# An attention and mixture-of-experts kernel: the second expert's weights move behind the first gathers, and the first value means come from a matmul

## The chip, the cores and the metric

The kernel runs on one core of a Trainium2 chip. The metric is the device time of one execution in microseconds (us), lower is better. TensorE, the matrix engine (PE in the profile), VectorE (DVE), ScalarE (ACT), GpSimd (POOL) and SyncE (SP) run their own instruction streams and wait for each other on semaphores. SP and POOL issue nearly all DMAs: SP's go through queue q1, POOL's through queue q0.

## The reference, cut to what matters

```python
# attention: B, H, S, D = 2, 8, 768, 64; block, window = 32, 16
k_sum = k.reshape(B, H, nb, block, D).max(axis=3)       # nb = 24 blocks
v_sum = v.reshape(B, H, nb, block, D).mean(axis=3)
# each query sees the keys less than 16 away, and 24 block maxima
# (their scores plus log(32)); softmax over both; values: v and v_sum
x = attention output as (1536, 512)
# mixture of experts: 8 experts, each token goes to its best two
for e in range(8):
    h = np.maximum(x[mask] @ w1[e], 0.0)        # w1[e]: 512 x 1024
    out[mask] += top2_w * (h @ w2[e])           # w2[e]: 1024 x 512
# then a dense layer: g = leaky(x @ w_in), g @ w_out, hidden width 2048
```

The block means of the values (`v_sum`) are what the change computes in another way for the first two heads. The two matrices of expert 1 are what it loads at another time.

## The kernel before, in words

**Attention.** Two heads make a pair; there are eight pairs (n = 0 to 7), each in three groups of four units of 64 queries (c = 3n + g). For a pair, SP loads the queries (L281), the keys (L285), the value windows with their two halos (L293 to L295) and the block means of the values (L302). PE transposes queries and keys into one shared bank, `turned` (L1044, L1053), and ACT and DVE copy them out (L612, L791, L617). For each group PE forms scores (L1066), DVE adds masks and takes maxima, ACT takes exponentials, PE transposes the probabilities (L1075) and multiplies them with the value windows (`weigh`, L1090), whose last 24 rows are the block means. Results go to the memory tensor `x_tokens` (L318).

**Block means.** For all heads they come from three loads of 128 rows of 8 KB (`load_rows`, L306) into the staging buffer `stage`, from five halving adds on POOL each (`block_means`, L465, L467), and from a store to memory (`store_means`, L311). `load_means` (L302) reads them back, broadcast over the twelve units. So the first `weigh` waits for rows, adds, a store and a load.

**SP** works through one hand-written list. A wait in it holds back every DMA that is written behind it.

**POOL** has one list too: constants, three `block_means`, the weights of expert 0, then (after the fifth transposed key pair) the weights of expert 1, a few constants, and the wait for the routing (`token_of_done`). `load_weights` brings one expert's two matrices in eight pieces of 512 KB through four slots of `stage` and splits each into a high and a low half (L495 and L497), 4 pieces for w1 (then `w1_ready`, L500) and 4 for w2 (then `w2_ready`). Two buffers of split weights exist: even experts use buffer 0, odd ones buffer 1.

**Routing.** Between attention and the experts, a chain mostly on DVE finds for each slot of each tile of 128 its token (`token_of`).

**Experts.** POOL gathers the token rows of tiles 0 to 2 straight into `x_first` (L548) and those of the others through a ring of seven slots into a memory tensor sorted by tile (gather L538, store L529, the store four tiles behind its gather). It gathers tiles up to 23, loads expert 2, gathers two tiles, loads expert 3, gathers the last five, and loads the others in a loop. PE runs the tiles in order: transposes, the second product of tile t-2, and the first product of tile t, which waits for `w1_ready` of its expert (L1190 is the matmul line of both products). After the experts comes the dense layer (L1274 to L1291).

Of the kernel before, what the change touches and what calls it, by code (L numbers as in the profile page):

```python
# [25 lines left out]
P = 128  # L26
# [9 lines left out]
KC = WK + NB  # L36
VC = D + 1
AT = P
MASKED = -1e9
EPS = 1e-9  # L40

# [25 lines left out]
def build(nc, q, k, v, w_gate, w_noise, noise, w1, w2, w_in, w_out, out):  # L67
    ctx = ExitStack()
    with ctx:
        def sem(name):  # L70
            return ctx.enter_context(nc.semaphore(name))

        def sb(name, shape, dt=F32, where=ctx):
            return where.enter_context(nc.sbuf_tensor(name, shape, dt))
# [32 lines left out]
        with ExitStack() as room:  # L107
            qk_nat = sb("qk_nat", [P, 2, TPB, 2, D], where=room)
            q_diag = sb("q_diag", [P, 2, UNITS, 2 * QB], where=room)
            kT = sb("kT", [P, 2, UNITS, KC], where=room)  # L110
            k_max = sb("k_max", [P, NB], where=room)
            v_win = sb("v_win", [KC, 2, 2, UNITS, VC], where=room)
            masks = sb("masks", [P, GROUPS - 1 + GU, KC], where=room)
            scores = sb("scores", [P, 2, GU, KC], where=room)
            probs = scores
            xT_gate = sb("xT_gate", [P, S], where=room)
            v_mean = xT_gate[:, 0:3 * D].rearrange("p (i d) -> p i d", i=3)
            negmax = sb("negmax", [P, 2, GU], where=room)
# [62 lines left out]
        zeros_done = sem("zeros_done")  # L181
# [39 lines left out]
        o_bank = [p67[:, 512 * i:512 * i + GU * VC].rearrange("x (u c) -> x u c", u=GU) for i in range(2)]  # L221
        gate_bank = [p67[:, 512 * i + GU * VC:512 * i + GU * VC + GM] for i in range(2)]
        last_gate_bank = p23[:, 0:GM]
        rank_bank = p01[:, 0:NT * E]
        count_bank = p23[:, 0:E]
        token_bank = p23[:, 512:512 + TCOLS]
# [51 lines left out]
        def _(sp):  # L278
# [24 lines left out]

            def load_rows(i):

                sp.dma_start(stage[:, 2 * (i % 2):2 * (i % 2) + 2, :].rearrange("p a n -> p (a n)"),  # L306
                             v_rows[i * P:(i + 1) * P, :]).then_inc(v_nat_loaded[i], 16)

            def store_means(i):
                sp.wait_ge(v_mean_done, i + 1)  # L310
                sp.dma_start(vsum_dram[i * P:(i + 1) * P, :], v_mean[:, i, :]).then_inc(v_mean_stored[i], 16)  # L311

            def store_x(n, g):

# [5 lines left out]

            load_q(0)
            load_k(0)
            load_rows(0)
            sp.wait_ge(consts_done, 2)
            load_windows(0)
            sp.wait_ge(q_turned, 1)
            load_q(1)
            sp.wait_ge(k_turned, 1)
            load_k(1)
            load_rows(1)  # L330
            sp.wait_ge(q_turned, 2)
            load_q(2)
            load_windows(1)
            store_means(0)
            load_rows(2)
            sp.wait_ge(v_mean_stored[0], 16)
            load_means(0)
            load_means(1)
            for n in range(PAIRS):
                if n + 2 < PAIRS:  # L340
                    sp.wait_ge(k_turned, n + 2)
                    load_k(n + 2)
                if n >= 1:
                    store_x(n - 1, 0)
                    if n + 1 < PAIRS:
                        sp.wait_ge(weighed, GROUPS * n)
                        load_windows(n + 1)
                        load_means(n + 1)
                    store_x(n - 1, 1)
                    store_x(n - 1, 2)  # L350
                if n + 3 < PAIRS:
                    sp.wait_ge(q_turned, n + 3)
                    load_q(n + 3)
                if n == 0:
                    for i in (1, 2):
                        store_means(i)
                    for i in (1, 2):
                        sp.wait_ge(v_mean_stored[i], 16)
            sp.wait_ge(k_turned, PAIRS)
            sp.dma_start(noise_sb[:], noise.rearrange("(t p) e -> p t e", p=P)).then_inc(noise_loaded, 16)  # L360
            for g in range(GROUPS):
# [56 lines left out]
        def _(pool):  # L418
# [20 lines left out]
            link(pool.memset(v_win[0:WINDOW, :, 0, 0, 0:D], 0.0))  # L439
            signal(pool.memset(v_win[64:WK, :, 1, UNITS - 1, 0:D], 0.0))  # L440

            link(pool.memset(masks[:, :, WK:KC], math.log(BLOCK)))
            link(pool.memset(masks[:, :, 0:WK], 0.0))
            units = GROUPS - 1 + GU
# [13 lines left out]

            def block_means(i):

                rows = stage[:, 2 * (i % 2):2 * (i % 2) + 2, :].rearrange("p a n -> p (a n)")
# [5 lines left out]
                pool.tensor_scalar(v_mean[:, i, :], rows[:, 0:D], 1.0 / BLOCK, 1.0, ALU.mult, ALU.mult).then_inc(v_mean_done, 1)  # L467

            def settled():

# [33 lines left out]
            pool.wait_ge(v_mean_done, 3)  # L504
            settled()
            load_weights(lambda c: weight_piece(0, c), 0, 0, reused=False)
            pool.wait_ge(k_turned, 5)
            load_weights(lambda c: weight_piece(1, c), 1, 1, reused=False)


            pool.wait_ge(k_turned, PAIRS)
# [78 lines left out]
        def _(act):  # L590
# [41 lines left out]
            q_part(0)  # L632
            k_part(0)
            k_means(0)
            q_part(1)
            for n in range(PAIRS):
                c = GROUPS * n
                if c >= 1:
                    probs_out(c - 1)
                softmax_exp(c)  # L640
                if n + 1 < PAIRS:
                    k_part(n + 1)

                probs_out(c)
                softmax_exp(c + 1)
                if n >= 2:
                    if n == 2:
                        for i in range(3):
                            act.wait_ge(v_mean_stored[i], 16)
                    act.wait_ge(gate_turned, n - 1)  # L650
                    act.wait_ge(gate_multiplied, n - 2)
                    gate_xT(n - 2)

                probs_out(c + 1)
                if n + 1 < PAIRS:
                    k_means(n + 1)
                softmax_exp(c + 2)
                if n + 2 < PAIRS:
                    q_part(n + 2)
# [77 lines left out]
        def _(dve):  # L737
# [70 lines left out]
            q_part(1)  # L808
            dve.wait_ge(consts_done, 3)
            for n in range(PAIRS):  # L810
                for g in range(GROUPS):
                    c = GROUPS * n + g
                    if c >= 3:
                        normalise(c - 3)
                    softmax_max(c)
                    if g == 1 and n + 1 < PAIRS:
# [14 lines left out]
            dve.wait_ge(consts_done, 5)  # L831
# [203 lines left out]
        def _(pe):  # L1035
# [42 lines left out]
            def weigh(c):  # L1078

                b = c % 2  # L1080
                n, g = divmod(c, GROUPS)
                if g == 0:
                    pe.wait_ge(v_loaded[n % 2], 80 * (n // 2 + 1))
# [12 lines left out]
            def gate_turn(m, first=0, end=TPB):  # L1096

# [19 lines left out]
            pe.wait_ge(zeros_done, 1)  # L1117
            turn_q(0)
            turn_k(0)
            turn_q(1)  # L1120
            for n in range(PAIRS):
                c = GROUPS * n
                score(c)
                if c >= 1:
                    turn_probs(c - 1)
                if n + 1 < PAIRS:
# [5 lines left out]
                turn_probs(c)  # L1132
                if n >= 2:
                    gate_turn(n - 2)
                if c >= 1:
# [205 lines left out]
```

## Time and profile before

| | |
|---|---|
| median of 3 runs | 835.51 us (832.05 to 835.52) |
| profiled execution | 829.91 us, its span 828.3 us |
| attention, to the last logits | 0 to 130.2 us of the span |
| routing | 130.2 to 153.1 us |
| first matmul of an expert | 159.26 us |
| last split of expert 1 | ends at 115.1 us |
| weight load of expert 2 | begins at 208.34 us |
| dense layer begins | about 550 us |

The times of the rows are microseconds from the start of the span, in one profiled execution. PE busy is the matrix engine's own busy time, PEclk its granted clock (1.00 is 2.4 GHz, 0.50 is 1.2 GHz), and the DMA share is that of 16 DMA engines.

### The profile page before, as it was taken

To read this page: it belongs to the slowest core of one execution; us is meant where nothing else is said; L and a number is where in the kernel's file an instruction comes from. 1 tells how busy PE (TensorE), PEld (TensorE's weight loads), DVE (VectorE), ACT (ScalarE), POOL (GpSimd) and SP (SyncE) were. 2 spreads that over 40 slices of the span, in tenths; PEclk is the share of its full clock that TensorE was granted. 3 is DMA by queue.
4 is the path that set the end of the run, shared out by engine and by line. 5 is a ranking of instruction groups with operands and counts; after the bars stand their busy time and mean duration, and the time that the engine had idled before them with its cause. 6 is when DMAs were issued, how large, how long until landed. Compare 5 with 4: busy or idle time off the path is not lost.

```text
span 828.3 us, 12304 instructions
## 1 busy us (share of the span) xinstructions
PE 754.7 (91%) x4026; PEld 632.2 (76%) x4027; DVE 272.5 (33%) x521; ACT 224.1 (27%) x405; POOL 392.5 (47%) x350
## 2 busy tenths in 40 slices
PE   3569892699999999999999999979999999999997
PEld 3458782578878888888888888878788887888885
DVE  3456556321221221222222122136343324432223
ACT  2557562022112212112112121225222222222221
POOL 5687860465786967888788783610011001000000
PEclk9889895599999999999999999989999999999999
DMA  9799970389726364353444441334011101010001
GB/s 213 177 286 227 268 128 13 112 288 297 242 89 215 127 214 173 120 187 143 144 142 156 138 141 38 114 127 154 13 39 51 51 1 50 0 51 0 0 1 51
DMA packets 87422, 103.15 MB, mean 125 GB/s; under 512 B 55680, under 2 KB 61824, under 8 KB 86976
## 3 DMA queue, kind: packets, MB, share of 16 engines
q0 software_dynamic: 17008, 59.52, 22.0%
q1 hardware_dynamic: 69328, 43.22, 20.5%
q8 instruction: 17, 0.28, 0.2%
q10 hardware_dynamic: 1056, 0.03, 0.1%
q14 instruction: 13, 0.11, 0.0%
HBM read 80.89 MB, written 23.69 MB: 126 GB/s over the span
## 4 chain that ended last, share of the span: by engine, by line
PE 61%; POOL 13%; DMA 10%; SPq 7%; DVE 4%; issue 4%; ACT 1%; POOLq 0%; DVEq 0%
PE p L1190 23%; POOL w_lo L497 6%; PE p L1274 5%; PE p L1276 5%; PE p L1275 5%; PE p L1289 5%; PE p L1291 5%; PE p L1290 5%; DMA x_by_tile<-x_ring 3%; POOL w_hi L495 3%; SPq L294 2%; DMA x_ring<-x_tokens,token_of 2%; POOL x_ring L538 2%; PE p L1182 2%; DMA stage<-in_moe_w 2%
## 5 line engine op out<-in xcount | busy, mean ns | idle before, releaser
L497 POOL TENSOR_TENSOR w_lo<-stage,w_hi 128x1024 fp32r<-128x1024 f32 x72 | 171.8, 2386 | 6.0
L1190 PE MATMUL p<-w_hi,xT_hi 128*128 x248 | 100.1, 404 | 3.3 <-DVE xT_lo L929 1.6
L584 POOL DMA_INDIRECT y_pick<-y_by_tile,slots x20 | 19.1, 955 | 165.9 <-PE p L1261 150.2
L1190 PE MATMUL p<-w_lo,xT_hi 128*128 x248 | 97.2, 392 | 0.0
L1190 PE MATMUL p<-w_hi,xT_lo 128*128 x248 | 97.2, 392 | 0.0
L1190 PE MATMUL p<-w_hi,hT_hi 128*128 x240 | 96.5, 402 | 0.0
L1190 PE MATMUL p<-w_lo,hT_hi 128*128 x240 | 93.9, 391 | 0.0
L1190 PE MATMUL p<-w_hi,hT_lo 128*128 x240 | 93.5, 390 | 0.0
L495 POOL TENSOR_SCALAR w_hi<-stage 128x1024 fp32r<-128x1024 f32 x72 | 75.9, 1054 | 18.9 <-DMA stage<-in_moe_w 14.8
L1274 PE MATMUL p<-f_xT_hi,w_hi 128*128 (+2 forms) x200 | 78.3, 392 | 1.3 <-DVE f_xT_lo L978 1.3
L1275 PE MATMUL p<-f_xT_lo,w_hi 128*128 (+2 forms) x200 | 77.2, 386 | 0.0
L1276 PE MATMUL p<-f_xT_hi,w_lo 128*128 (+2 forms) x200 | 77.1, 386 | 0.0
L1289 PE MATMUL p<-w_hi,f_hT_hi 128*128 128x512 f32 x192 | 75.0, 390 | 1.4 <-DVE f_hT_lo L988 1.3
L1291 PE MATMUL p<-w_hi,f_hT_lo 128*128 128x512 f32 x192 | 74.7, 389 | 0.0
L1290 PE MATMUL p<-w_lo,f_hT_hi 128*128 128x512 f32 x192 | 74.7, 389 | 0.0
L686 ACT CAST hT_hi<-p 128x1024 fp32r<-128x1024 f32 x30 | 30.5, 1015 | 156.5 <-PE p L1182 143.3
L929 DVE TENSOR_TENSOR xT_lo<-p,xT_hi 128x512 fp32r<-128x512 f32 x31 | 21.4, 692 | 154.6 <-ACT xT_hi L683 149.9
L986 DVE SCALAR_TENSOR_TENSOR f_h<-p,f_h 128x512 f32<-128x512 f32 x48 | 33.2, 691 | 116.6 <-ACT f_h L708 116.6
L681 ACT ACTIVATE h_row<-p 128x1024 f32<-128x1024 f32 x30 | 30.8, 1027 | 139.7 <-PE p L1190 134.6
L708 ACT COPY f_h<-p 128x512 f32<-128x512 f32 x48 | 28.2, 588 | 142.2 <-PE p L1276 142.2
L935 DVE COPY y_row<-p 128x512 f32<-128x512 f32 x31 | 21.5, 693 | 115.6 <-PE p L1190 115.6
L476 POOL DMA_DIRECT2D stage<-in_moe_w x64 | 41.5, 650 | 33.0 <-POOL w_lo L497 22.5
(184 smaller groups left out, 1253.8 us busy)
## 6 DMA issues: line engine op xcount, KB each, us to landing
stage<-in_moe_w POOLq DMA_DIRECT2D x64, 512.0 KB, 4.9
y_by_tile<-y_row SPq DMA_DIRECT2D x31, 256.0 KB
x_by_tile<-x_ring POOLq DMA_DIRECT2D x28, 256.0 KB, 6.9
x_row<-x_by_tile SPq DMA_DIRECT2D x28, 256.0 KB
qk_nat<-in_q SPq DMA_DIRECT2D x16, 192.0 KB, 5.6
qk_nat<-in_k SPq DMA_DIRECT2D x16, 192.0 KB, 4.7
stage<-in_v SPq DMA_DIRECT2D x3, 1024.0 KB, 7.8
v_win<-in_v SPq DMA_DIRECT2D x8, 384.0 KB
```

The source lines that it names most:

```text
L476: pool.dma_start(stage_view(c % STAGES, c), source(c)).then_inc(staged[c % STAGES], 16)
L495: pool.tensor_scalar(w_hi[:, par, cols], stage[:, c % STAGES, :], 1.0, 1.0, ALU.mult, ALU.mult).then_inc(hi_split, 1)
L497: pool.tensor_tensor(w_lo[:, par, cols], stage[:, c % STAGES, :], w_hi[:, par, cols].bitcast(F32), ALU.subtract).then_inc(lo_split, 1)
L681: nc.scalar.activation(h_row[:], h_bank[:], ACT.Relu).then_inc(h_ready, 1)
L986: nc.vector.scalar_tensor_tensor(out=h, in0=f_h_bank[c % 2], scalar=0.01, in1=h, op0=ALU.mult, op1=ALU.max).then_inc(f_leaky_done, 1)
L1190: last = nc.tensor.matmul(bank, a, w, start=(c == 0 and i == 0), stop=(c == left_hi.shape[1] - 1 and i == 2))
L1274: nc.tensor.matmul(to, hi, f_xT_hi[:, cols], start=(k == 0), stop=False)
L1275: nc.tensor.matmul(to, hi, f_xT_lo[:, cols], start=False, stop=False)
L1276: last = nc.tensor.matmul(to, lo, f_xT_hi[:, cols], start=False, stop=(k == KD - 1))
L1289: nc.tensor.matmul(f_y_bank[m], f_hT_hi[:, c % 2, rows], hi, start=(c == 0), stop=False)
L1290: nc.tensor.matmul(f_y_bank[m], f_hT_hi[:, c % 2, rows], lo, start=False, stop=False)
L1291: last = nc.tensor.matmul(f_y_bank[m], f_hT_lo[:, c % 2, rows], hi, start=False, stop=(c == FC - 1))
```

## The change

1. The weights of expert 1 are loaded (and split) after the gathers of tiles 0 to 9, and no longer during attention. The gathers of tiles 10 to 23 and everything that POOL does after them come behind that load.
2. The block means of the first pair (`n = 0`) come from twelve accumulating matmuls of a 0-or-1/32 matrix (`in_block`) with the value windows, and one ScalarE copy that broadcasts them into the window tile. The first 48 rows of means are no longer summed on POOL, and `load_means(0)` is gone. The three row loads are now of 128, 128 and 80 rows (`MEAN_ROWS`).
3. The order of the first loads on SP and of the first turns on PE, ACT and DVE: the second pair's queries turn after the first scores, its keys after the first probabilities; row loads 1 and 2 come later, and the stores of means 1 and 2 (with SP's waits for them) move into the later rounds of the loop, ahead of `load_means(n + 1)`.

```diff
+MEAN_ROWS = [(2 * NB, 2 * NB + P), (2 * NB + P, 2 * NB + 2 * P), (2 * NB + 2 * P, B * H * NB)]
...
 (SyncE)
             load_q(0)
             load_k(0)
-            load_rows(0)
             sp.wait_ge(consts_done, 2)
             load_windows(0)
             sp.wait_ge(q_turned, 1)
             load_q(1)
+            load_rows(0)
             sp.wait_ge(k_turned, 1)
             load_k(1)
-            load_rows(1)
+            load_windows(1)
             sp.wait_ge(q_turned, 2)
             load_q(2)
-            load_windows(1)
             store_means(0)
-            load_rows(2)
+            load_rows(1)
             sp.wait_ge(v_mean_stored[0], 16)
-            load_means(0)
             load_means(1)
             for n in range(PAIRS):
...
+                if n == 0:
+                    load_rows(2)
...
                         load_windows(n + 1)
+                        if n < 3:
+                            store_means(n)
+                            sp.wait_ge(v_mean_stored[n], 16)
                         load_means(n + 1)
...
-                if n == 0:
-                    for i in (1, 2):
-                        store_means(i)
-                    for i in (1, 2):
-                        sp.wait_ge(v_mean_stored[i], 16)
...
 (GpSimd)
+            link(pool.memset(in_block[:], 0.0))
+            blocks = in_block[:, NB - 2:NB]
+            link(pool.memset(blocks, 1.0 / BLOCK))
+            link(pool.affine_select(out=blocks, ...))
+            signal(pool.affine_select(out=blocks, ...))
...
             load_weights(lambda c: weight_piece(0, c), 0, 0, reused=False)
-            pool.wait_ge(k_turned, 5)
-            load_weights(lambda c: weight_piece(1, c), 1, 1, reused=False)
...
-            gather_tiles(FIRST, 2 * NT)
+            gather_tiles(FIRST, FIRST + RING)
+            load_weights(lambda c: weight_piece(1, c), 1, 1, reused=False)
+            gather_tiles(FIRST + RING, 2 * NT)
             pool.wait_ge(table_done, 1)
             load_weights(lambda c: weight_piece(2, c), 2, 0)
...
 (ScalarE, after softmax_exp(0))
+                if n == 0:
+                    act.wait_ge(first_means_done, 1)
+                    nc.scalar.copy(v_win[WK:KC, 0, :, :, 0:D], first_mean_bank ... broadcast over UNITS).then_inc(first_means_ready, 1)
+                    q_part(1)
...
 (TensorE)
+            def first_means():
+
+                pe.wait_ge(v_loaded[0], 48)
+                pe.wait_ge(consts_done, 3)
+                for u in range(UNITS):
+                    last = nc.tensor.matmul(first_mean_bank, in_block[:, NB - 2 - 2 * u:2 * NB - 2 - 2 * u], v_win[0:WK, 0, :, u, 0:D],
+                                            start=(u == 0), stop=(u == UNITS - 1))
+                last.then_inc(first_means_done, 1)
...
             turn_q(0)
             turn_k(0)
-            turn_q(1)
             for n in range(PAIRS):
                 c = GROUPS * n
                 score(c)
...
-                if n + 1 < PAIRS:
+                if n == 0:
+                    first_means()
+                    turn_q(1)
+                elif n + 1 < PAIRS:
                     turn_k(n + 1)
...
                 score(c + 1)
                 turn_probs(c)
+                if n == 0:
+                    turn_k(1)
```

## Rows read from the trace of the kernel before

**Rows 1.** The page, busy time of the engines over the span.
```profile
PE 754.7 (91%) x4026; PEld 632.2 (76%) x4027; DVE 272.5 (33%) x521; ACT 224.1 (27%) x405; POOL 392.5 (47%) x350
```
**Rows 2.** Busy time by stretch: stretch, length, engines, then clock, DMA share, GB/s.
```profile
0.00:130.20 130.20, 92.68 (x912) 82.52 (x913) 66.78 (x148) 67.87 (x155) 88.07 (x93) 0.91 0.96 209
...
230.40:330.50 100.10, 98.75 (x484) 81.97 (x482) 21.16 (x25) 20.45 (x25) 77.19 (x63) 1.00 0.48 163
330.50:828.30 497.80, 485.16 (x2264) 402.55 (x2264) 151.00 (x236) 117.74 (x203) 174.68 (x135) 0.99 0.24 80
```
**Rows 3.** Timeline of PE, first products of tiles 0, 3, 6, 14; start, duration.
```profile
159.26 0.79 PE L1190 MATMUL p<-w_hi,xT_hi 128*128 x1 [1.60 <-DVE xT_lo L929]
...
162.69 0.40 PE L1190 MATMUL p<-w_lo,xT_hi 128*128 x1
...
193.58 0.48 PE L1190 MATMUL p<-w_hi,xT_hi 128*128 x1
...
231.74 0.49 PE L1190 MATMUL p<-w_hi,xT_hi 128*128 x1 [1.00 <-POOLq L500]
...
330.50 0.49 PE L1190 MATMUL p<-w_hi,xT_hi 128*128 x1 [0.35 <-POOLq L500]
```
**Rows 4.** Timeline of POOL, from the first gather to the load of expert 2.
```profile
153.09 1.06 POOL L548 DMA_INDIRECT x_first<-x_tokens,token_of  x1 [36.26 <-DVE token_of L925]
...
165.75 0.98 POOL L538 DMA_INDIRECT x_ring<-x_tokens,token_of  x1 [0.30 <-issue]
...
167.62 0.98 POOL L538 DMA_INDIRECT x_ring<-x_tokens,token_of  x1 [0.30 <-issue]
...
193.05 0.97 POOL L538 DMA_INDIRECT x_ring<-x_tokens,token_of  x1 [4.89 <-DMA x_by_tile<-x_ring]
...
200.77 0.97 POOL L538 DMA_INDIRECT x_ring<-x_tokens,token_of  x1 [0.30 <-DMA x_by_tile<-x_ring]
...
208.34 1.60 POOL L476 DMA_DIRECT2D stage<-in_moe_w  x3
```
**Rows 5.** Groups of POOL instructions, 150 to 210 us: count, busy, mean; idle before.
```profile
L538 POOL DMA_INDIRECT x_ring<-x_tokens,token_of x21 | 20.3, 967 | 15.4 <-DMA x_by_tile<-x_ring 10.8 <-issue 4.6
L529 POOL DMA_DIRECT2D x_by_tile<-x_ring x21 | 12.2, 580 | 3.8 <-DMA x_ring<-x_tokens,token_of 3.8
```
**Rows 6.** Timeline of POOL: ends of expert 1's load, and of expert 2's.
```profile
76.07 2.19 POOL L476 DMA_DIRECT2D stage<-in_moe_w  x4 [0.61 <-POOL w_lo L497]
...
112.77 2.36 POOL L497 TENSOR_TENSOR w_lo<-stage,w_hi 128x1024 fp32r<-128x1024 f32 x1
...
229.09 2.37 POOL L497 TENSOR_TENSOR w_lo<-stage,w_hi 128x1024 fp32r<-128x1024 f32 x1
...
247.90 1.06 POOL L538 DMA_INDIRECT x_ring<-x_tokens,token_of  x1 [0.83 <-POOL w_lo L497]
```
**Rows 7.** DMA queues in 0:102.5, then 76:102.5 (two rows), then 37:50: packets, MB, share.
```profile
q1 hardware_dynamic: 48427, 15.98, 80.1%
...
q1 hardware_dynamic: 12639, 3.54, 77.7%
q0 software_dynamic: 1016, 3.70, 40.7%
...
q1 hardware_dynamic: 3926, 1.05, 42.2%
```
**Rows 8.** The chain that ended last, in time: the last key load.
```profile
95.34 7.16 DMA qk_nat<-in_k
```
**Rows 9.** Timeline of PE in attention: turn, first product with values, scores.
```profile
16.25 1.54 PE L1044 MATMUL p<-ident,qk_nat 128*128 128x128 f32 x6 [7.23 <-DMA qk_nat<-in_q]
...
32.41 1.19 PE L1090 MATMUL p<-v_win,probsT 120*64 120x65 f32 x16 [6.30 <-DMA v_win<-v_means]
...
69.29 1.15 PE L1066 MATMUL p<-kT,q_diag 128*128 128x120 f32 x8
...
79.61 1.15 PE L1066 MATMUL p<-kT,q_diag 128*128 128x120 f32 x8
```

More of the change, by code:

```diff
@@ L117, in build @@
             v_mean = xT_gate[:, 0:3 * D].rearrange("p (i d) -> p i d", i=3)
+            in_block = xT_gate[0:WK, 3 * D:3 * D + 2 * NB - 2]
             negmax = sb("negmax", [P, 2, GU], where=room)
@@ L180, in build @@
         v_loaded = [sem(f"v_loaded{i}") for i in range(2)]
-        zeros_done = sem("zeros_done")
+        zeros_done = sem("zeros_done"); first_means_done = sem("first_means_done"); first_means_ready = sem("first_means_ready")
         q_turned = sem("q_turned"); k_turned = sem("k_turned")
@@ L223, in build @@
         last_gate_bank = p23[:, 0:GM]
+        first_mean_bank = p67[WK:KC, 512:512 + 2 * D]
         rank_bank = p01[:, 0:NT * E]
@@ L304, in load_rows @@
             def load_rows(i):
-                sp.dma_start(stage[:, 2 * (i % 2):2 * (i % 2) + 2, :].rearrange("p a n -> p (a n)"),
-                             v_rows[i * P:(i + 1) * P, :]).then_inc(v_nat_loaded[i], 16)
+                first, end = MEAN_ROWS[i]
+                sp.dma_start(stage[0:end - first, 2 * (i % 2):2 * (i % 2) + 2, :].rearrange("p a n -> p (a n)"),
+                             v_rows[first:end, :]).then_inc(v_nat_loaded[i], 16)
             def store_means(i):
+                first, end = MEAN_ROWS[i]
                 sp.wait_ge(v_mean_done, i + 1)
-                sp.dma_start(vsum_dram[i * P:(i + 1) * P, :], v_mean[:, i, :]).then_inc(v_mean_stored[i], 16)
+                sp.dma_start(vsum_dram[first:end, :], v_mean[0:end - first, i, :]).then_inc(v_mean_stored[i], 16)
             def store_x(n, g):
@@ L440, in _ @@
             signal(pool.memset(v_win[64:WK, :, 1, UNITS - 1, 0:D], 0.0))
+            link(pool.memset(in_block[:], 0.0))
+            blocks = in_block[:, NB - 2:NB]
+            link(pool.memset(blocks, 1.0 / BLOCK))
+            link(pool.affine_select(out=blocks, in_=blocks, compare_op=ALU.is_ge, fill=0.0, base=-WINDOW, pattern=[[-BLOCK, 2]], channel_multiplier=1))
+            signal(pool.affine_select(out=blocks, in_=blocks, compare_op=ALU.is_ge, fill=0.0, base=WINDOW + BLOCK - 1, pattern=[[BLOCK, 2]], channel_multiplier=-1))
             link(pool.memset(masks[:, :, WK:KC], math.log(BLOCK)))
@@ L459, in block_means @@
             def block_means(i):
-                rows = stage[:, 2 * (i % 2):2 * (i % 2) + 2, :].rearrange("p a n -> p (a n)")
+                first, end = MEAN_ROWS[i]
+                rows = stage[0:end - first, 2 * (i % 2):2 * (i % 2) + 2, :].rearrange("p a n -> p (a n)")
                 pool.wait_ge(v_nat_loaded[i], 16)
@@ L466, in block_means @@
                     half //= 2
-                pool.tensor_scalar(v_mean[:, i, :], rows[:, 0:D], 1.0 / BLOCK, 1.0, ALU.mult, ALU.mult).then_inc(v_mean_done, 1)
+                pool.tensor_scalar(v_mean[0:end - first, i, :], rows[:, 0:D], 1.0 / BLOCK, 1.0, ALU.mult, ALU.mult).then_inc(v_mean_done, 1)
             def settled():
@@ L634, in _ @@
             k_means(0)
-            q_part(1)
             for n in range(PAIRS):
@@ L640, in _ @@
                 softmax_exp(c)
-                if n + 1 < PAIRS:
+                if n == 0:
+                    act.wait_ge(first_means_done, 1)
+                    nc.scalar.copy(v_win[WK:KC, 0, :, :, 0:D], first_mean_bank.rearrange("x (h d) -> x h d", h=2).unsqueeze(2).to_broadcast([NB, 2, UNITS, D])).then_inc(first_means_ready, 1)
+                    q_part(1)
+                elif n + 1 < PAIRS:
                     k_part(n + 1)
@@ L645, in _ @@
                 softmax_exp(c + 1)
+                if n == 0:
+                    k_part(1)
                 if n >= 2:
@@ L807, in _ @@
             k_blocks(0)
-            q_part(1)
-            dve.wait_ge(consts_done, 3)
+            dve.wait_ge(consts_done, 4)
             for n in range(PAIRS):
@@ L815, in _ @@
                     softmax_max(c)
-                    if g == 1 and n + 1 < PAIRS:
+                    if c == 0:
+                        q_part(1)
+                    if c == 2:
+                        k_blocks(1)
+                    if g == 1 and 1 <= n < PAIRS - 1:
                         k_blocks(n + 1)
@@ L830, in _ @@
             dve.wait_ge(noise_loaded, 16)
-            dve.wait_ge(consts_done, 5)
+            dve.wait_ge(consts_done, 6)
             dve.wait_ge(logits_added, PAIRS + 1)
@@ L1081, in weigh @@
                 n, g = divmod(c, GROUPS)
-                if g == 0:
-                    pe.wait_ge(v_loaded[n % 2], 80 * (n // 2 + 1))
+                if c == 0:
+                    pe.wait_ge(first_means_ready, 1)
+                if g == 0 and n >= 1:
+                    pe.wait_ge(v_loaded[n % 2], (80 if n % 2 else 48) + 80 * (n // 2))
                 pe.wait_ge(probsT_ready, c + 1)
@@ L1125, in _ @@
                     turn_probs(c - 1)
-                if n + 1 < PAIRS:
+                if n == 0:
+                    first_means()
+                    turn_q(1)
+                elif n + 1 < PAIRS:
                     turn_k(n + 1)
@@ L1132, in _ @@
                 turn_probs(c)
+                if n == 0:
+                    turn_k(1)
                 if n >= 2:
```

## The prediction

> **What bounds the kernel now.** I read the page first: PE is busy 91% of the span, POOL 47% [rows 1]. That average hides three stages, so I went on to the busy time by stretch. In attention, the first 130.2 us, PE is busy 92.7 us; the DMA share is 0.96 [rows 2]. From 230.4 us on PE has almost no gap: 98.75 of 100.1 us, then 485.2 of 497.8 us, the gaps of the latter being in the dense layer [rows 2]. Whatever delays PE at about 230 us therefore delays the end by the same amount; nothing later takes it up.
>
> Next the timeline of PE at the start of each expert. The first product of tile 6 starts at 231.74 us, after 1.00 us of waiting for POOL's L500, the signal that an expert's w1 is split; tile 14 waits 0.35 us at 330.50 us for the same line [rows 3]. So tile 6 is the first of expert 2 (POOL's load that ends its fourth split at 229.09 + 2.37 = 231.5 us is the one begun at 208.34 us [rows 4, 6]). Experts 0 and 1 have six tiles, and POOL's chain (gathers, expert 2, expert 3, expert 4) is exactly as long as PE's, with no slack at all at two places. That is the fact on which the forecast rests: **work added to POOL between 153 and 208 us is work added to the end.**
>
> In attention the question is what ends the waits. The chain that ended last runs through SP's DMAs and their landings up to the last key load, 95.34 + 7.16 = 102.5 us [rows 8]; from there 27.7 us remain to 130.2. Up to 102.5 us q1 is busy 80.1%, 82.1 us [rows 7]: attention is paced mainly by SP's queue of small packets.
>
> **The load of expert 1 behind the gathers.** I follow POOL from its first gather, 153.09 us, in times of before.
>
> Block one, the gathers of tiles 0 to 9: the last starts at 165.75 us [rows 4], 12.7 us in. Then its remaining stores must wait for their gathers to land. The same tail before, from the last gather at 200.77 us to the load at 208.34, is 7.6 us [rows 4]. Sum 20.2 us.
>
> The load itself: from 208.34 to the next gather at 247.90 us, 39.6 us [rows 4, 6]; in attention expert 1 took 76.07 to 115.13, 39.1 us [rows 6]. POOL splits in order, so none of this lies beside other POOL work. I take 39.6, with up to 41.0 if DMA is crowded.
>
> Block two, the gathers of tiles 10 to 23: before, from 167.62 to 208.34, 40.7 us [rows 4]. Four of the stores in it (tiles 6 to 9, 0.58 us each [rows 5]) now belong to block one: 38.4. It held ring waits: 10.8 us in six, against 0.3 us that every gather has, 9.0 us too much; one was 4.89 us [rows 4, 5]. After the load the ring is empty, and a gather meets its slot's store three gathers after it was issued. I keep three waits of 1.2 us, 3.5 us: 32.9 us. Low: no ring waits; high: all of them, 38.4. The tail waits (3.8 us [rows 5]) may partly go in both blocks, 2.2 us each at the low end.
>
> Sum: 20.2 + 39.6 + 32.9 = 92.7 us, against 208.34 - 153.09 = 55.3 before. Expert 2's load starts **37.5 us later** against the end of routing; low 18.0 + 39.6 + 27.2 = 84.8 (+29.6), high 20.2 + 41.0 + 38.4 = 99.6 (+44.4).
>
> What is late next: the first product of tile 3, the first of expert 1, stands at 193.58 us [rows 3]; its w1 would be ready 23.2 us (208.34 to 231.5) after 173.3, at 196.5, so PE waits 3 us there. The wait at tile 6 swallows it: PE is ready at about 234 and starts at 269, some 35 us idle. From there POOL needs 122.2 us from expert 2's load to expert 4's w1, as before (208.34 to 330.5), and PE needs its eight tiles of 12.3 us [rows 3] too, so the delay neither grows nor shrinks. The clock adds a little: after the idle of routing the first eight matmuls took 159.26 to 162.69, 3.4 us, instead of the 1.8 that they take at the pace of a tile, 48 products and twelve short transposes in 12.3 us, some 0.23 us each [rows 3]. The idle at tile 6 should cost the same 1.6 us, less the 0.6 us by which tile 14 was late anyway: **+1.0 us**. Bounds 0 and 2.
>
> **What attention gives back.** In 76 to 102.5 us, with expert 1's weights beside it, q1 is busy 77.7%, idle 5.9 us [rows 7]. Without those weights I give that back in full: 5.9. The 576 packets of `load_means(0)` at 82.1 x 16 / 48427 = 27.1 ns are 1.0 us of the 16 engines; the 48 rows not loaded, 0.39 MB, are about 1.2 us at the rate of 0.96 DMA share [rows 2, 7]. Sum 2.2. The hole from 37 to 50 us, where q1 is busy only 42.2%, 7.5 us idle [rows 7], comes where SP stands at the stores of means 1 and 2 before it loads keys; these now come later, but SP now stands at `store_means(0)` for the same sums and meets the others in rounds 1 and 2, each ahead of `load_means` and of a whole round of loads. I count half, 3.8. Together **G = 12 us**.
>
> The early waits, 7.23 us for queries before the first scores and 6.30 us for `v_means` before the first `weigh` [rows 9], both go; but they are waits on the queue that paces the whole stage, and taking them away only lets PE reach the next load sooner. They are not added. The new matmuls cost under 1.2 us (16 of L1090 took 1.19 [rows 9]) and the copy little more, hidden by the loads of pair 1. The four small POOL constants are hidden by the wait for the first rows. PE now waits for windows 0 before it turns the second queries, and behind that stand the keys of pair 1; between 0 and 5 us if those windows are late.
>
> Bounds of G: at most q1 without gaps, 82.1 - 2.2 + 2.3 of start = 82.2 instead of 102.5: 20.3. At least 0.
>
> A rule speaks to the 5.9. The Trainium skill, DMA: Bandwidth & Descriptors, section Queues, rings and completion order, says that each DMA engine takes turns between the queue rows that have work, a packet at a time. Then each weight packet held q1 back by its own time, 40.7% of 26.5 us = 10.8 us [rows 7], where the idle share gives 5.9; by it G is 16.9 and the time 5 us less.
>
> **The sum.** 829.9 (the profiled execution; its span is 828.3) + 37.5 + 1.0 - 12 = 856.4. The median of the runs, 835.5, stands 5.6 above that execution; the middle of all four times is 832.7, and with +26.5 it gives **859 us**.
>
> **Rivals.**
> - **Attention gives more back**, G from 15 to 20: the turns between queues, or the hole goes fully. For it: the 10.8 us above. Against it: it needs an SP that stands nowhere, and each round has waits for `weighed` and `x_ready` in front of the next windows. Time with G = 17 to 20: 851 to 854. Chance 0.18.
> - **The change does not do what it says in attention**, G under 7: SP stands behind the sums of means, or behind the windows, and the freed DMA time is idle. For it: the hole at 37 to 50 us is of this kind and is only moved. Time with G = 2: 869. Chance 0.14.
> - **Not slower**, through one mechanism: q1's price per packet falls once the weights are gone. With q1 gapless (G = 20.3) a further 18 us are needed, 48427 packets falling from 27.1 to 21 ns. In 37 to 50 us they took 5.5 x 16 / 3926 = 22.4 ns [rows 7], but those were another mix. At 20 ns G is 42 and the time 829. Against it too: attention would have to end at about 92 us, with PE busy for 92.7 [rows 2], while an undisturbed pair takes 79.61 - 69.29 = 10.3 us [rows 9]. Faster 0.04, same 0.02.
>
> My forecast's own case (G 7 to 15) has 0.62. The range: with G = 20.3 and +29.6 it would be 843, with G = 5 and +44.4 it would be 873; both ends at once are unlikely, so 847 to 870. What this measurement can tell from no change is about 0.5%, 4 us. Slower: 0.94.
>
> **What would show it.** PE idle of 30 to 40 us before tile 6's first product, put down to L500, and PEclk at half there; POOL's eight splits of expert 1 between the gathers; the routing's end about 12 us earlier, near 141 us; q1 above 85% from 76 us on; the first scores at about 12 us. I would be wrong if PE's wait at tile 6 were under 25 us (block two much quicker), or if routing ended before 130 us.

## The result and the profile after

The changed kernel takes **867.3 us** (median of 4 runs, 863.5 to 869.0) against 835.5 (832.1 to 837.2): a ratio of 1.038, 95% interval 1.033 to 1.043. It is slower, by 31.8 us in the medians. The profiled execution took 863.45 us, its span 861.9, which is 33.6 more than the span before.

The page after, busy time and its 40 slices (21.5 us each), then the group that POOL holds up:

```profile
PE 758.8 (88%) x4050; PEld 634.3 (74%) x4051; DVE 272.7 (32%) x521; ACT 225.2 (26%) x406; POOL 393.8 (46%) x354
...
PE   5829973889707999999999999988999999999997
...
PEclk9869985899957999999999999998999999999999
...
L1223 PE MATMUL p<-w_hi,xT_hi 128*128 x248 | 101.6, 410 | 38.1 <-POOLq L510 36.1
```

PE has only 4.1 us more to do than in [rows 1], but its share falls from 91 to 88%. The twelfth slice (237 to 259 us), an idle PE at half its clock, is the one to explain: it lies just ahead of expert 2's tiles. The same by stage (columns as in [rows 2]):

```profile
0.00:125.50 125.50, 93.49 (x936) 82.15 (x937) 66.82 (x148) 69.02 (x156) 56.37 (x73) 0.90 0.91 179
125.50:148.40 22.90, 6.87 (x30) 6.55 (x30) 19.49 (x97) 3.35 (x5) 0.00 (x0) 0.50 0.00 1
148.40:264.30 115.90, 73.51 (x340) 60.01 (x340) 15.65 (x18) 15.68 (x19) 85.94 (x84) 0.81 0.64 211
264.30:365.00 100.70, 100.67 (x484) 83.81 (x485) 19.66 (x23) 19.73 (x24) 76.62 (x63) 0.98 0.49 159
365.00:861.90 496.90, 484.22 (x2262) 401.82 (x2260) 151.03 (x236) 117.47 (x203) 174.82 (x135) 0.99 0.24 80
```

The last two stretches stand for the last two of [rows 2] and are within 1 us of them. All of the loss is in the third: from the end of routing to tile 6 it was 231.74 - 153.09 = 78.65 us, and is 115.9 now. Attention gives 4.65 us back. PE's waits, summed, name the two places:

```profile
PE p L1223 <- POOLq L510: 36.1, 2, 32.8
PE p L1062 <- ACT xT_gate L637: 15.4, 1, 15.4
...
PE p L1062 <- DMA qk_nat<-in_q: 4.9, 1, 4.9
```

Columns: total, times, longest. The first row is the forecast wait (L510 is the old L500, L1223 the old L1190). The second was not forecast.

**POOL, where the forecast lay.** Its timeline, to be held against [rows 4] and [rows 6]:

```profile
148.44 1.06 POOL L556 DMA_INDIRECT x_first<-x_tokens,token_of  x1 [47.97 <-DVE token_of L943]
...
161.08 0.99 POOL L546 DMA_INDIRECT x_ring<-x_tokens,token_of  x1 [0.30 <-issue]
...
168.33 2.13 POOL L486 DMA_DIRECT2D stage<-in_moe_w  x4
...
208.97 1.07 POOL L546 DMA_INDIRECT x_ring<-x_tokens,token_of  x1 [0.79 <-POOL w_lo L507]
...
239.13 1.61 POOL L486 DMA_DIRECT2D stage<-in_moe_w  x3
...
261.71 2.34 POOL L507 TENSOR_TENSOR w_lo<-stage,w_hi 128x1024 fp32r<-128x1024 f32 x1
```

Block one is 148.44 to 168.33 = 19.9 us, the load 40.6, block two 30.2; together 90.7 against 55.25 before: +35.4. Expert 2's first weights then take 24.9 us to `w1_ready` (23.2 before). PE's timeline:

```profile
192.98 0.79 PE L1223 MATMUL p<-w_hi,xT_hi 128*128 x1 [3.35 <-POOLq L510]
...
264.33 0.79 PE L1223 MATMUL p<-w_hi,xT_hi 128*128 x1 [32.79 <-POOLq L510]
...
267.86 0.40 PE L1223 MATMUL p<-w_lo,xT_hi 128*128 x1
```

Tile 3 waits 3.35 us and tile 6 32.79 us; the next eight products take 3.5 us instead of 1.8, at a granted clock of 0.51, the lower of the two levels. That is [rows 3] moved by 37.2 us against the end of routing.

**Attention, where it did not lie.** SP and then ScalarE at the second wait:

```profile
53.91 0.47 SPq L298 DMA_DIRECT2D v_win<-in_v  x1
54.42 0.46 SPq L316 DMA_DIRECT2D v_means<-xT_gate  x1
61.43 0.76 SPq L305 DMA_DIRECT2D v_win<-v_means  x2
```

```profile
61.55 0.80 ACT L637 COPY xT_gate<-p 128x768 f32<-128x768 f32 x1 [15.78 <-issue]
```

The sums of means (`v_mean`) lie in the memory of `xT_gate`. So before ScalarE writes the first `xT_gate` it waits for all three stores of means. The third store stands in round 2 of SP's list now, behind the windows of the next pair and what those wait for; it is issued at 54.42, and SP's wait for its landing ends by 61.4. Until then ScalarE stands for 15.8 us and PE for 15.4. The idle is labelled "issue" on ScalarE: only the code and SP's timeline say what it was.

### The profile page after: what moved, and what is told of

Its sections match the earlier page's. It is cut to its first block, busy times and chain, and to the rows that moved or that the text cites. A ratio compares the mean times of both kernels' runs of the same rounds, so it can differ in the third digit from the quotient of the medians.

```text
span 861.9 us, 12355 instructions
## 1 busy us (share of the span) xinstructions
PE 758.8 (88%) x4050; PEld 634.3 (74%) x4051; DVE 272.7 (32%) x521; ACT 225.2 (26%) x406; POOL 393.8 (46%) x354
## 3 DMA queue, kind: packets, MB, share of 16 engines
q0 software_dynamic: 17008, 59.52, 21.5%
q1 hardware_dynamic: 68632, 42.66, 19.9%
## 4 chain that ended last, share of the span: by engine, by line
PE 74%; POOL 8%; DMA 7%; issue 4%; DVE 4%; ACT 1%; SPq 1%; DVEq 0%; POOLq 0%; ACTq 0%
PE p L1223 33%; PE p L1307 5%; PE p L1308 5%; PE p L1309 5%; PE p L1322 5%; PE p L1323 5%; PE p L1324 5%; POOL w_lo L507 3%; PE p L1215 3%; PE p L1084 2%; DMA x_by_tile<-x_ring 2%; PE p L1110 2%; POOL w_hi L505 1%; POOL x_ring L546 1%; DMA stage<-in_moe_w 1%
## 5 line engine op out<-in xcount | busy, mean ns | idle before, releaser
L1223 PE MATMUL p<-w_hi,xT_hi 128*128 x248 | 101.6, 410 | 38.1 <-POOLq L510 36.1
L1223 PE MATMUL p<-w_hi,xT_lo 128*128 x248 | 98.5, 397 | 0.0
L1223 PE MATMUL p<-w_lo,xT_hi 128*128 x248 | 98.3, 396 | 0.0
L1223 PE MATMUL p<-w_hi,hT_hi 128*128 x240 | 96.5, 402 | 0.0
L1223 PE MATMUL p<-w_lo,hT_hi 128*128 x240 | 93.9, 391 | 0.0
L1223 PE MATMUL p<-w_hi,hT_lo 128*128 x240 | 93.5, 390 | 0.0
L505 POOL TENSOR_SCALAR w_hi<-stage 128x1024 fp32r<-128x1024 f32 x72 | 76.0, 1056 | 24.7 <-DMA stage<-in_moe_w 19.8
L1223 PEld LDWEIGHTS p<-w_hi,xT_hi 128*128 128x128 f32 x248 | 47.9, 193 | 48.3 <-issue 39.2
L953 DVE COPY y_row<-p 128x512 f32<-128x512 f32 x31 | 21.5, 694 | 117.1 <-PE p L1223 107.4
```

The costliest lines, as they stand in the source:

```text
L505: pool.tensor_scalar(w_hi[:, par, cols], stage[:, c % STAGES, :], 1.0, 1.0, ALU.mult, ALU.mult).then_inc(hi_split, 1)
L1223: last = nc.tensor.matmul(bank, a, w, start=(c == 0 and i == 0), stop=(c == left_hi.shape[1] - 1 and i == 2))
```

## The experiments

Ratios are against the kernel before on the same chip. "Lead" is how much earlier than 153.09 us POOL's first gather starts in the profiled execution: what attention and routing gave back. Each lead comes from one execution of each kernel. The changed kernel and gathers_later are the same up to there, and their first gathers start at 148.44 and 147.79 us; the last logits of half_behind and late_gap_old_order, also the same up to there, come at 121.71 and 124.80. A lead is therefore good to some 3 us.

### The load alone (move_only)

```diff
-            pool.wait_ge(k_turned, 5)
-            load_weights(lambda c: weight_piece(1, c), 1, 1, reused=False)
...
-            gather_tiles(FIRST, 2 * NT)
+            gather_tiles(FIRST, FIRST + RING)
+            load_weights(lambda c: weight_piece(1, c), 1, 1, reused=False)
+            gather_tiles(FIRST + RING, 2 * NT)
```

> The kernel before with one edit: expert 1's weights load between the gathers of tiles 9 and 10, and no longer in attention. First theory (POOL's chain is the delay): tile 6 starts about 37 us later after the end of routing than before (115 to 117 us after the first gather instead of 78.7), attention ends 4 to 8 us earlier, and the kernel takes 28 to 34 us more than before, ratio 1.033 to 1.041. Rival (the loss comes from the new order of the first loads and turns, the weights only fill gaps of POOL): ratio within 1.01 of before, and PE waits under 5 us for L500 at tile 6.

Measured: 859.3 us, ratio 1.032 (1.025 to 1.039). Lead 8.7 us (first gather at 144.41), longest wait for the split weights 33.0 us. The load's move alone gives nearly the whole loss (1.032 of 1.038, with intervals that overlap), and without the new order attention gives back more, not less.

### The new order and the matmul means alone (order_only)

The changed kernel, with expert 1's load again in attention, behind `k_turned` 5.

> The changed kernel with expert 1's load put back into attention, behind the fifth key turn: only the matmul means and the new order are left. First theory: no wait at tile 6 beyond the 1 us of before; ScalarE's wait for the stored means (15.8 us in the changed kernel) is still there and eats what the faster start gives, so attention ends between 122 and 130 us and the ratio to before is 0.99 to 1.00. Rival (the new order itself costs time): attention ends after 132 us, ratio over 1.003.

Measured: 837.7 us, ratio 1.007 (1.003 to 1.010). Lead -5.2 us: routing ends later than before. The wait for `xT_gate` is there, 15.8 us, with the third store issued at 56.55. The new order is a loss by itself; the rival was right.

### The third store right behind the second (stores_together)

```diff
-                        if n < 3:
-                            store_means(n)
-                            sp.wait_ge(v_mean_stored[n], 16)
+                        if n == 1:
+                            store_means(1)
+                            store_means(2)
+                            sp.wait_ge(v_mean_stored[1], 16)
+                        if n == 2:
+                            sp.wait_ge(v_mean_stored[2], 16)
```

> The changed kernel with one edit: the third store of means is issued right behind the second, one round earlier than in the changed kernel. First theory (ScalarE's copy of xT_gate stands 15.8 us for that store, and PE behind it): the wait of PE for xT_gate falls under 2 us, attention ends 8 to 15 us earlier than in the changed kernel (111 to 118 us), and the time is 852 to 860, ratio to before 1.020 to 1.030. Rival (the DMA queue paces attention, the wait only shows where): the 15 us turn up as waits for queries and keys, and the time stays within 4 us of the changed kernel, ratio 1.034 to 1.042.

Measured: 858.6 us, ratio 1.031 (1.024 to 1.037). The wait for `xT_gate` is gone, lead 9.8 us instead of 4.65. Its waits of PE:

```profile
PE p L1226 <- POOLq L513: 33.7, 2, 30.9
PE p L1065 <- DMA qk_nat<-in_q: 12.7, 3, 5.4
```

A stall of 15.4 us was worth 5.1 of lead; 7.8 of the rest came back as waits for queries (12.7 instead of 4.9), on the queue that paces attention. Where the last 2.5 went is not shown. The ratio alone does not tell this kernel from the change: the two intervals overlap.

### The same repair with the load in attention (order_fixed)

order_only, with the stores as in stores_together.

> The new order and the matmul means with the third store one round earlier, and expert 1's load in attention as before. Theory (the order alone cost 5 us through ScalarE's wait for the stored means): attention ends at 125 to 131 us against 135.4 with that wait and 130.2 before; ratio 0.992 to 1.002. Rival (the DMA queue takes back all that is gained): attention ends at 133 us or later, ratio 1.005 or more.

Measured: 831.4 us, ratio 0.999 (0.995 to 1.002); lead 2.0 us; tile 6 waits 0.7 us. The repair is worth 7.2 us of lead here, and the intervals of order_only and order_fixed do not overlap: the store's place is a loss of its own. With it mended the new order and the matmul means neither gain nor lose by what this measurement can tell.

### The load in POOL's idle time ahead of the routing's end (fix_gap)

stores_together, with expert 1's load behind the last constants and ahead of `pool.wait_ge(token_of_done, 1)`, where POOL stands idle for 48 us in the changed kernel.

> The previous kernel with expert 1's load moved once more: behind the last key turn and POOL's last constants, ahead of its wait for the routing, where POOL stands idle 48 us in the changed kernel. First theory: the load (40 us) ends before or within 3 us of the end of routing, tile 6 starts 78 to 80 us after the first gather again, and the whole gain of attention reaches the end: 815 to 823 us, ratio 0.975 to 0.987. Rival (POOL's splits slow VectorE's routing chain, or the load ends after it): routing takes over 26 us instead of 22.9, or the first gather waits for POOL over 5 us, ratio 0.99 or more.

Measured: 831.6 us, ratio 1.000 (0.996 to 1.003). The load started at 98.50 us, beside the last windows and means, which it held up. PE at the last pair, and the queues in 98 to 110 us:

```profile
117.25 1.19 PE L1112 MATMUL p<-v_win,probsT 120*64 120x65 f32 x16 [4.82 <-DMA v_win<-v_means]
```

```profile
q0 software_dynamic: 605, 2.22, 54.0%
q1 hardware_dynamic: 2714, 0.80, 46.2%
```

The last logits came at 133.97 us, 13.8 later than in stores_together (120.17), and the lead is -4.6 us. The wait of 4.8 us is only the start of it: PE was idle for much of 110 to 117 us, and its clock fell for the rest of attention, where stores_together had 1.00:

```profile
117.20:134.00 16.80, 15.46 (x100) 13.84 (x100) 2.53 (x12) 2.34 (x4) 15.67 (x11) 0.50 0.35 102
```

Tile 6 waits 2.9 us. This profiled execution took 837.2 us, the longest of ten with a median of 831.6, so -4.6 overstates the usual loss; what the others did no trace shows. By the median the kernel is back where the kernel before was: the load's move no longer costs, and attention's gain does not reach the end.

### The same, but behind the last windows (late_gap, late_gap_old_order)

```diff
+            pool.wait_ge(v_loaded[1], 80 * (PAIRS // 2))
+            load_weights(lambda c: weight_piece(1, c), 1, 1, reused=False)
             pool.wait_ge(token_of_done, 1)
```

late_gap is stores_together with this, late_gap_old_order the kernel before with it; in both, expert 1's load stands only there.

> The kernel with the stores together (third store of means one round earlier) and expert 1's load in POOL's idle time, now gated on the landing of the last pair's value windows and means, not on the last key turn. Theory (in the previous kernel the weights held back the last pair's means, 4.8 us of waiting and then a slow clock): the wait for v_means is gone, attention ends at 119 to 123 us as with the stores together, the load runs from about 109 to 149 us and overruns the end of routing by 4 to 7 us; first gather at 147 to 150 us against 153.1 before, no wait at tile 6 over 3 us, ratio to before 0.990 to 0.998. Rival (POOL's splits or weights beside routing slow it down anyway): first gather after 152 us, ratio 0.999 or more.

> The kernel before with one edit: expert 1's load moved into POOL's idle time, gated on the landing of the last pair's windows and means. Theory: attention ends at 120 to 124 us, as when the load was moved behind the gathers (121.5), first gather at 147 to 151 us, ratio 0.991 to 0.999, within 0.004 of the same kernel with the new order: the new order is worth next to nothing. Rival (the new order and the matmul means are worth 5 us or more once their stall is mended): this one is slower than that one by over 0.006.

Measured: 836.9 us, ratio 1.005 (1.001 to 1.008), and 838.2 us, ratio 1.006 (1.003 to 1.008). The two differ by 0.001, so the new order with its stall mended is worth too little to be seen here as well. Attention kept its gain (last logits at 119.92 in late_gap), but the first gather starts at 158.05: routing takes 38 us instead of 22.9. The stretch of routing in late_gap:

```profile
119.90:158.10 38.20, 6.86 (x30) 6.54 (x30) 35.24 (x97) 3.34 (x5) 22.64 (x16) 0.50 0.13 42
```

DVE runs the same 97 instructions as in the changed kernel, but is busy for 35.2 us instead of 19.5, and POOL is busy for 22.6 where it was idle. Side by side in late_gap:

```profile
139.12 2.46 DVE L885 TENSOR_TENSOR r_sc<-chosen 128x96 f32<-128x96 f32 x1
...
142.66 2.21 DVE L887 COPY r_sc<-r_sc 128x8 f32<-128x8 f32 x1
```

```profile
139.06 2.34 POOL L510 TENSOR_TENSOR w_lo<-stage,w_hi 128x1024 fp32r<-128x1024 f32 x1
141.37 1.05 POOL L508 TENSOR_SCALAR w_hi<-stage 128x1024 fp32r<-128x1024 f32 x1
142.50 2.34 POOL L510 TENSOR_TENSOR w_lo<-stage,w_hi 128x1024 fp32r<-128x1024 f32 x1
```

and the same two DVE operations in the kernel before:

```profile
138.44 0.32 DVE L864 TENSOR_TENSOR r_sc<-chosen 128x96 f32<-128x96 f32 x1
...
139.19 0.17 DVE L866 COPY r_sc<-r_sc 128x8 f32<-128x8 f32 x1
```

Both DVE operations end when POOL's subtraction ends (139.12 + 2.46 = 141.6 beside 139.06 + 2.34 = 141.4; 142.66 + 2.21 = 144.9 beside 142.50 + 2.34 = 144.8). It is not the weights' DMAs that hold them, for none was under way here (the last two figures are the DMA share and GB/s):

```profile
137.80:145.00 7.20, 0.00 (x0) 0.02 (x1) 7.06 (x6) 0.00 (x0) 6.87 (x5) 0.50 0.00 0
```

Nor does every DVE operation stand. The searches for the best experts ran at their usual 0.16 us beside another subtraction:

```profile
132.09 2.34 POOL L510 TENSOR_TENSOR w_lo<-stage,w_hi 128x1024 fp32r<-128x1024 f32 x1
```

```profile
133.18 0.16 DVE L876 FIND_INDEX8 top_at<-top,r_sc 128x8 uint32<-128x8 f32 x1
```

### Only 8 of the 1024 columns split (gap_short_split, after_short_split)

```diff
-                    cols = slice(c * CW, (c + 1) * CW)
+                    width = 8 if isinstance(e, int) and e == 1 else CW
+                    cols = slice(c * CW, c * CW + width)
```

`stage` is read at that width too. All DMAs are kept. Left out is the split of the other 1016 columns: instead POOL copies expert 0's split weights into the second buffer once, in attention, so expert 1's products have other values. The first kernel is late_gap with this, the second the changed kernel with it. The copies are not free: in the second they take 14 us of POOL, and its first gather starts at 151.89 instead of 148.44.

> The kernel with the late gap (stores together, expert 1's load gated on the last pair's windows), but of each piece of expert 1 only 8 of 1024 columns are split; all its DMAs stay. (POOL copies expert 0's split weights into the buffer once, in its idle time before the gate, so the values of expert 1's tiles are not the reference's.) Theory (VectorE's routing chain stands behind POOL's two-input subtraction of 2.3 us each time): with the subtractions gone, the first gather follows the last logits by 22.9 to 24 us as before, against 37.9 us with the full split. Rival (the weights' DMAs beside routing slow it, or the noise and x_tokens transfers come late): still over 30 us.

> The changed kernel, but of each piece of expert 1 only 8 of 1024 columns are split; all its DMAs and waits stay. (Again POOL copies expert 0's split weights into the buffer once in attention, and the values are not the reference's.) Theory (POOL's own time for the split, 28 us, is what delays expert 2): the load behind the gathers takes 14 to 22 us instead of 40.6, and PE's wait for L510 at tile 6 falls from 32.8 to 7 to 15 us; the span is 16 to 26 us shorter than the changed kernel's. Rival (the DMAs of the weights among gathers and stores are what takes the time): the load still takes over 32 us.

Measured, one run each: 822.5 us and 850.6 us. In the first the routing takes 22.4 us again (last logits 123.21, first gather 145.83): without POOL's long splits DVE is not slowed. Of the DMAs this run says little, since without the splits they ran ahead and flowed beside only the first 2 us of routing; the empty DMA stretch in late_gap above is what rules them out.

In the second the load takes 24.7 us instead of 40.6, tile 6 starts 99.9 us after the first gather instead of 115.9, and still waits 20 us:

```profile
251.75 0.79 PE L1226 MATMUL p<-w_hi,xT_hi 128*128 x1 [19.96 <-POOLq L511]
```

Neither expectation holds: the first wanted 14 to 22 us of load, a wait of 7 to 15 and a span shorter by 16 to 26 (it is 13.0), the rival over 32 us of load. POOL's groups from 172.0 to 196.8 us show what is left:

```profile
L506 POOL TENSOR_SCALAR w_hi<-stage 128x8 fp32r<-128x8 f32 x8 | 1.6, 204 | 12.3 <-DMA stage<-in_moe_w 12.2
```

With the splits gone POOL waits for weights to land, 12.2 us. So at 40.6 us the load is paced by the splits, with a DMA time of about 25 us hidden under them: a faster split alone could take back 16 us, not 40 (an estimate: 40.6 - 24.7).

### Half of the load behind the gathers (half_behind)

The kernel before, with w1 of expert 1 in the idle time (behind the last windows) and w2 between the gathers of tiles 9 and 10, three of its four pieces fetched before them.

> The kernel before with expert 1's load split: its first matrix (4 pieces) in POOL's idle time, gated on the last pair's windows, its second (4 pieces, 3 of them fetched early) between the gathers of tiles 9 and 10. Theory (each us of POOL work between the end of routing and expert 2's load is a us at the end): expert 2's load starts 66 to 69 us after the first gather (55.3 before, 90.7 in the changed kernel), tile 6 waits 10 to 14 us, ratio to before 1.001 to 1.010. Rival (it is the late w1 of expert 1 that delays PE, at tile 3): with w1 early there is no wait at tile 6 over 3 us, ratio under 0.998.

Measured: 843.4 us, ratio 1.012 (1.008 to 1.017). The load of expert 2 starts 65.8 us after the first gather (55.3 before, 90.7 after the change), and tile 6 waits 12 us:

```profile
241.37 0.79 PE L1191 MATMUL p<-w_hi,xT_hi 128*128 x1 [11.95 <-POOLq L502]
```

So half of the load adds 10.5 us to POOL's list where the whole adds 35.4, and the wait is about a third of 32.8; the splits of w1 beside the routing made that 29.5 us long. The ratio is just above the 1.001 to 1.010 expected.

### Gathers of tiles 10 to 23 behind expert 2's load (gathers_later)

The changed kernel, with `load_weights` of expert 2 ahead of `gather_tiles(FIRST + RING, 2 * NT)`.

> The changed kernel with the gathers of tiles 10 to 23 behind expert 2's load instead of ahead of it, nothing else. Theory (POOL's list up to expert 4's w1 is as long as PE's, so 37 us of added work come out at tile 14 wherever the gathers stand): tile 6 starts about 29 us earlier against the first gather (84 to 88 us), but PE then waits over 20 us at tile 10, and the first product of tile 14 starts 213 to 216 us after the first gather as in the changed kernel; ratio to before 1.031 to 1.043. Rival (only the wait at tile 6 counts, the rest has slack): ratio 1.000 to 1.012.

Measured: 861.0 us, ratio 1.036 (1.029 to 1.042), an interval that overlaps that of the change itself. Tile 6 starts 82.4 us after the first gather without a wait, but:

```profile
305.00 0.79 PE L1222 MATMUL p<-w_hi,xT_hi 128*128 x1 [24.82 <-POOLq L510]
...
357.35 0.49 PE L1222 MATMUL p<-w_hi,xT_hi 128*128 x1 [1.24 <-POOLq L510]
```

The wait is at tile 10 instead. Tile 14 starts 357.35 - 147.79 = 209.6 us after the first gather, against 364.12 - 148.44 = 215.7 after the change and 177.4 before. POOL's work up to expert 4 is what counts; its order moves the place of the wait and 6 us of its size. The expectation was right in kind, but both places came earlier than it said (84 to 88 and 213 to 216).

## Why the prediction was right, and where it was not

| step of the prediction | forecast | measured |
|---|---|---|
| block one, load, block two | 20.2 + 39.6 + 32.9 = 92.7 | 19.9 + 40.6 + 30.2 = 90.7 |
| expert 2's load begins, against the end of routing | +37.5 | +35.4 |
| expert 2's w1 ready, against the same | +37.5, with its 23.2 us unchanged | +37.2 |
| wait of tile 3 | 3 | 3.35 |
| idle ahead of tile 6 | about 35 | 32.79 |
| lost from tile 6 to tile 14, by the clock | +1.0 | +1.0 (38.27 - 37.24) |
| first scores | about 12 us | 11.84 |
| q1's share from 76 us on | above 85% | 114.8% |
| G, what attention gives back | 12 | 4.65 |
| end of routing | near 141 us | 148.4 us |
| time | 859 (847 to 870) | 867.3 |

**Right: the bound.** The claim that work added to POOL between 153 and 208 us is work added to the end held in all runs. The load moved alone gives it (1.032), half of it gives less (1.012), a cheaper split takes 16 us off the stretch from the first gather to tile 6 (13 off the span), and another order moves it to another tile. With the load put back, or in POOL's idle time, tile 6 waits 0.7 to 2.9 us. The working had one shift within it: block two was 2.7 us shorter than its term (its waits for the ring and at the tail were shorter), while the first piece of expert 2 came later, 24.9 us to ready instead of 23.2.

**Wrong: the size of G.** Forecast 859 against 867.3: 7.35 of the 8.3 us are G. That 867.3 still lies in the stated range, 847 to 870, is owed to the range's width and not to the working of attention. The case that held was the second rival, "the change does not do what it says in attention", to which I gave 0.14. I had named its place too (SP stands behind the sums of means), but not its mechanism. And one of the signs of being right failed: routing was to end about 12 us earlier, and ended 4.65 earlier. The runs split G into its two parts, each to be read with the 3 us of doubt of a lead:

| | forecast | measured (lead) |
|---|---|---|
| no weights beside attention | 5.9 | 8.7 (move_only) |
| new order and matmul means | 2.2 + 3.8 | -5.2 (order_only); 2.0 with the stores together |
| both | 12 | 4.65; 9.8 with the stores together |

The steps that failed are these. (1) "these now come later, but SP now stands at `store_means(0)` for the same sums", with half of the hole counted as a gain of 3.8. I asked only what SP's own wait holds back. The third store also holds back ScalarE, since the sums lie in `xT_gate`, and through it PE: 15.4 us that the kernel before did not have. Undoing it adds 5.1 us of lead (to 9.8, within the forecast's own case) or, with the load in attention, 7.2 (to 2.0). (2) Even mended, the order gives 2.0 rather than 6.0. The hole did close in part: in 37 to 50 us after,

```profile
q1 hardware_dynamic: 4784, 1.32, 62.0%
```

where it was 42.2%, some 2.6 us of the 13 more, against the 3.8 counted. But in order_fixed PE still stands for the same queue, 16.6 us in four waits:

```profile
PE p L1065 <- DMA qk_nat<-in_q: 16.6, 4, 5.2
```

Before it was 21.6 us in five waits for queries and 6.3 for means: 11 us of waiting are gone, and 2.0 of lead came of it. The prediction said of the early waits that their end gives nothing by itself, and left them out of the sum; it should have said it of the hole. One more price in it was too low: the new matmuls took 3.5 us in the changed kernel, not under 1.2. And the 48 rows that are no longer loaded were mispriced: 0.39 MB at 209 GB/s and a share of 0.96 [rows 2] are 1.8 us, not 1.2. Neither is large, and what they did to the end no run separates. (3) The weights' own term was probably too small. By the idle share I gave 5.9; the packets' own time in [rows 7] gave 10.8; 8.7 were measured, between the two.

On (3), the queues after the change, in 76 to 98.1 us:

```profile
q1 hardware_dynamic: 14365, 3.97, 114.8%
```

Before, q1 and q0 together stood at 77.7 + 40.7 = 118.4% [rows 7]; now q1 alone stands at 114.8%. So q1 took over nearly all of the weights' share, and moved 650 packets per us instead of 477. The Trainium skill, DMA: Bandwidth & Descriptors, section Queues, rings and completion order, says that each DMA engine takes turns between the queues, packet by packet. By that rule 10.8 us were to come back, and 8.7 did; with the 3 us of doubt of a lead, this run does not decide between it and the idle share. The bound of G at 20.3 was worked out as if a queue's share could not pass 100%; it can, so that number was no bound.

The rival "not slower" failed as forecast: no price of q1's packets fell (1.148 x 22.1 x 16 / 14365 = 28.3 ns after; 0.777 x 26.5 x 16 / 12639 = 26.1 before).

What stays open: why the repair is worth 7.2 us of lead with the load in attention and 5.1 without (within the doubt of a lead, so the difference may be nothing); why order_fixed gains so little from 11 us less waiting; and a version that keeps attention's gain without splitting beside the routing or behind the gathers. None of the kernels that compute all of the reference is faster than the one before by what can be measured; order_fixed at 0.999 and fix_gap at 1.000 come closest.

## What to carry to other kernels

Where an engine works through one list and another engine waits for its last item without slack, price a moved piece at its full length at the new place, whatever it frees at the old one. Before a store or a signal is moved, look for every tensor that shares its memory, and for who waits on it for that reason; the queue's own list shows only half of the waiters. And a stall beside a busy queue is not worth its whole length: here 15.4 us were worth 5 to 7. A trace shows one execution: before a lead is explained, see where that execution stands among the others.

## What the runs showed of the hardware

**Some DVE operations stand while GpSimd works.** While POOL ran its 2.34 us subtraction of two 128x1024 operands in late_gap, two short DVE operations took as long as it ran: a two-input one 2.46 us instead of 0.32, and a copy of 128x8 2.21 instead of 0.17. The index searches beside another such subtraction kept their 0.16 us. POOL's one-input copies of 1.05 to 1.15 us also held DVE: an operation at 138.11 us, beside one of them, took 0.97 us instead of 0.26. Over the routing this added 15 us to a chain of 22.9 us; with the splits cut to 8 columns it was gone. The Trainium skill, GPSIMD Engine Reference, section Key points, tells of contention with DVE instructions in a 2-port mode or with two SBUF inputs. The two-input row agrees. The copy has one input, and whether it ran in a 2-port mode no run here shows.

**A queue's share can pass 100% of the 16 engines' time** (114.8% above): so the times of some packets in the profile must overlap on the same engine, and a share is no utilisation with a ceiling.
